# Attention pairs before two gated layers: scores moved ahead of all transposes, a second probability buffer, and weight splitting moved up in GpSimd's queue

## What is computed

```python
B, H, S, D = 4, 8, 576, 64
scores = where(causal, -1e9, q @ k.T / sqrt(D));  a = softmax(scores);  local = a @ v
q_p = phi(q)                                   # phi(x) = x > 0 ? x + 1 : exp(x)
mem_out = (q_p @ M_prev) / (q_p @ z_prev + 1e-6)
attn = g * mem_out + (1 - g) * local           # g = sigmoid(beta) by head
x = attn as 2304 tokens x 512
h = x @ w_in;  x = act(h) @ w_out              # 512 -> 2048 -> 512, piecewise quadratic gate
h = x @ w_in2; out = (h * sigmoid(h)) @ w_out2 # 512 -> 2048 -> 512
```

## Time and profile before

| | us |
|---|---|
| median of 3 runs | 986.52 (985.75 to 989.36) |
| the profiled execution | 986.77 |
| its span, first to last instruction | 984.6 |
| TensorE busy | 974.2 (99%) |
| VectorE, ScalarE, GpSimd busy | 478.4, 384.0, 286.0 |

### The profile page before, as it was taken

The page is one execution under the profiler, slowest core; times in us unless marked ns, Lnnn a source line. Parts: engine busy times, 40 slices in busy tenths (PEclk is TensorE's granted clock), DMA queues, the critical chain, the costliest instruction groups (busy, mean ns, idle before and its releaser), DMA issues.

```text
span 984.6 us, 14130 instructions
## 1 busy us (share of the span) xinstructions
PE 974.2 (99%) x5468; PEld 814.4 (83%) x5468; DVE 478.4 (49%) x946; ACT 384.0 (39%) x847; POOL 286.0 (29%) x304
## 2 busy tenths in 40 slices
PE   8999999999999999999999999999999999999998
PEld 6888778888888888888888998888888888888897
DVE  7999999756344434434344663323332332322232
ACT  7988888633223222322223332322222232222222
POOL 7999999799000000000000798000000000000000
PEclk9999999999999999999999999999999999999999
DMA  6555454244000000000000343001000100100010
GB/s 213 152 161 157 145 145 141 60 128 117 12 1 1 1 0 1 1 1 1 1 1 1 87 133 92 0 1 43 1 1 1 44 0 1 43 1 1 1 44 22
DMA packets 38401, 48.10 MB, mean 49 GB/s; under 512 B 3264, under 2 KB 21696, under 8 KB 38336
## 3 DMA queue, kind: packets, MB, share of 16 engines
q1 hardware_dynamic: 38336, 47.20, 16.0%
HBM read 42.47 MB, written 4.72 MB: 48 GB/s over the span
## 4 chain that ended last, share of the span: by engine, by line
PE 89%; DVE 6%; ACT 2%; issue 1%; DMA 0%; POOL 0%; SPq 0%; POOLq 0%
PE ps L1020 26%; PE ps L1022 26%; PE ps L1021 26%; PE ps L953 3%; PE ps L898 3%; PE ps L861 2%; DVE prob L652 1%; PE ps L973 1%; PE ps L877 1%; DVE glo L796 1%; ACT prob L475 1%; DVE qlo L634 1%; DVE rw L684 1%; PE ps L939 1%; PE ps L946 1%
## 5 line engine op out<-in xcount | busy, mean ns | idle before, releaser
L1020 PE MATMUL ps<-xhi,W 128*128 128x512 f32 (+1 forms) x640 | 235.5, 368 | 0.0
L1021 PE MATMUL ps<-xlo,W 128*128 128x512 f32 (+1 forms) x640 | 235.4, 368 | 0.0
L1022 PE MATMUL ps<-xhi,W 128*128 128x512 f32 (+1 forms) x640 | 235.4, 368 | 0.0
L796 DVE TENSOR_TENSOR glo<-act_t,ghi 128x512 fp32r<-128x512 f32 (+1 forms) x160 | 118.1, 738 | 223.5 <-ACT ghi L575 223.5
L575 ACT CAST ghi<-act_t 128x512 fp32r<-128x512 f32 (+1 forms) x160 | 92.5, 578 | 235.4 <-PE ps L1022 213.1
L1020 PEld LDWEIGHTS ps<-xhi,W 128*128 128x128 f32 x640 | 120.6, 188 | 20.7
L1021 PEld LDWEIGHTS ps<-xlo,W 128*128 128x128 f32 x640 | 120.6, 188 | 20.6
L1022 PEld LDWEIGHTS ps<-xhi,W 128*128 128x128 f32 x640 | 120.6, 188 | 20.0
L335 POOL CAST W<-stage 128x512 fp32r<-128x512 f32 x64 | 49.1, 767 | 303.0 <-PE ps L1022 300.6
L567 ACT ACTIVATE act_t<-act_t,half_col 128x512 f32<-128x512 f32 (+1 forms) x80 | 54.5, 681 | 185.7 <-DVE act_t L789 185.7
L1020 PE MATMUL ps<-ghi,W 128*128 128x512 f32 (+1 forms) x320 | 118.1, 369 | 0.2
(11 more groups left out here) (113 smaller groups left out, 1334.9 us busy)
## 6 DMA issues: line engine op xcount, KB each, us to landing
stage<-in_moe_w_in SPq DMA_DIRECT2D x32, 256.0 KB, 2.7
stage<-in_moe_w_out SPq DMA_DIRECT2D x32, 256.0 KB, 2.7
vn<-in_vN SPq DMA_DIRECT2D x16, 320.0 KB, 4.5
qraw<-in_qT SPq DMA_DIRECT2D x15, 320.0 KB, 3.4
qn<-in_qN SPq DMA_DIRECT2D x16, 288.0 KB, 4.1
zb<-in_zN SPq DMA_DIRECT2D x32, 144.0 KB, 3.8
out_x<-ostage SPq DMA_DIRECT2D x17, 256.0 KB, 2.0
kraw<-in_kT SPq DMA_DIRECT2D x15, 288.0 KB, 3.0
```

Of the source, the lines that this page charges most:

```text
L796: nc.vector.tensor_tensor(glo[:, f % SLOTS, 0:TN[tile]], a, ghi[:, f % SLOTS, 0:TN[tile]].bitcast(F32), ALU.subtract).then_inc(glo_done, 1)
L1020: nc.tensor.matmul(dst, w_lo_, x_hi_, start=first, stop=False)
L1021: nc.tensor.matmul(dst, w_hi_, x_lo_, start=False, stop=False)
L1022: return nc.tensor.matmul(dst, w_hi_, x_hi_, start=False, stop=last)
```

## The change

In its turn p (from p = 1 on) TensorE takes the four score blocks of pair p+1 first, straight behind the value products of pair p-1, and then all transposes of pair p. `prob` has two buffers, chosen by p % 2, so the maxima of pair p+1 need not wait until the blocks of pair p are turned. T_M0 is turned into bank 0, T_M30 into bank 1, T_M21 into bank 0 after T_M0 is emptied. VectorE's turn starts with `to_x(p-1)` and maxima 0 to 3, and only then has `rows(p)` and `empty_second(p)`. ScalarE makes the feature rows and three exponentials ahead of T_M0. GpSimd has `split_part` behind `widen(p)` and ahead of `phi_sum_2(p+1)`.

```diff
@@ -82,7 +82,7 @@
         phs = sb("phs", [P, NB + 1, D], where=att)
         vn = sb("vn", [P, 2, FULL + 1, 2, D], where=att)
         mb = sb("mb", [P, 2, P], where=att)
-        prob = sb("prob", [P, 2, tri(FULL) * P], where=att)
+        prob = sb("prob", [P, 2, 2, tri(FULL) * P], where=att)
         ptail = sb("ptail", [P, MAIN + P], where=att)
         probT = sb("probT", [P, 2, FULL + 1, S], where=att)
         turned = sb("turned", [P, 2, S], where=att)
...
@@ -430,6 +431,9 @@
                 weigh(p)
                 widen(p)
 
+                for u in parts_beside(p):
+                    split_part(u)
+
                 if 0 < p < NPAIR - 1:
                     phi_sum_2(p + 1)
                 if p + 2 < NPAIR:
...
@@ -438,8 +442,6 @@
                 if p + 1 < NPAIR:
                     phi_times_z(p + 1)
                     weigh_v(p + 1)
-                for u in parts_beside(p):
-                    split_part(u)
             for u in range(2 * EARLY, 4 * FC):
                 split_part(u)
 
...
@@ -521,27 +523,30 @@
                 more = p + 1 < NPAIR
 
                 made_here = p + 2 if p else 1
+                if p == 0:
+                    phi_part_1(1)
+                    empty_main(0, T_M20, 2, 0)
+                    empty_main(0, T_M30, 3, 0)
+                    phi_part_2(1)
+                elif made_here < NPAIR:
+                    phi_part_1(made_here)
+                    phi_part_2(made_here)
+                if more:
+                    for c in range(3):
+                        exps(p + 1, c)
                 if p:
                     empty_first(p)
-                if made_here < NPAIR:
-                    phi_part_1(made_here)
-                empty_main(p, T_M20, 2, 0)
-                if p == 0:
-                    empty_main(0, T_M30, 3, 0)
-                if made_here < NPAIR:
-                    phi_part_2(made_here)
                 if more:
-                    exps(p + 1, 0)
-                    exps(p + 1, 1)
+                    exps(p + 1, 3)
                 if p:
+                    empty_main(p, T_M20, 2, 0)
                     empty_main(p, T_M30, 3, 0)
-                if more:
-                    exps(p + 1, 2)
-                    exps(p + 1, 3)
+                if p and more:
+                    exps(p + 1, 4)
                 empty_main(p, T_M31, 3, 1)
                 empty_tail(p)
-                if more:
-                    exps(p + 1, 4)
+                if p == 0:
+                    exps(1, 4)
                 empty_rest(p)
                 empty_phi(p)
                 empty_row(p)
...
@@ -733,18 +734,17 @@
             dve.wait_ge(made, 14)
             for p in range(NPAIR):
                 more, more2 = p + 1 < NPAIR, p + 2 < NPAIR
+                if p and more:
+                    to_x(p - 1)
+                if more:
+                    for c in range(4):
+                        maximum(p + 1, c)
                 if p:
                     for step in range(4):
                         rows(p, step)
-                    if more:
-                        to_x(p - 1)
-                        empty_second(p)
-                    else:
-                        empty_second(p)
-                        to_x(p - 1)
-                if more:
-                    for c in range(4):
-                        maximum(p + 1, c)
+                    empty_second(p)
+                if not more:
+                    to_x(p - 1)
                 if p == 0:
                     norms(0, 0)
                     norms(0, 1)
...
@@ -850,8 +850,8 @@
                     pe.wait_ge(lo_done, 2 * p + 2)
                     if p:
                         pe.wait_ge(s_read, NB * p)
-                if s == 2 and p:
-                    pe.wait_ge(ev_act, len(BY_ACT) * (p - 1) + BY_ACT.index(T_M0) + 1)
+                if s == 2 and p == 1:
+                    pe.wait_ge(ev_act, BY_ACT.index(T_M0) + 1)
                 if s == 3:
                     pe.wait_ge(x_free, p)
                 for part, (a, b_) in enumerate(three_of):
...
@@ -868,9 +868,9 @@
                 if half == 0:
                     pe.wait_ge(s_read, NB * p + 4)
                     if p:
-                        pe.wait_ge(ev_act, len(BY_ACT) * (p - 1) + BY_ACT.index(T_M30) + 1)
+                        pe.wait_ge(ev_dve, len(BY_DVE) * (p - 1) + BY_DVE.index(T_M21) + 1)
                 elif p:
-                    pe.wait_ge(ev_dve, len(BY_DVE) * (p - 1) + BY_DVE.index(T_M21) + 1)
+                    pe.wait_ge(ev_act, len(BY_ACT) * (p - 1) + BY_ACT.index(T_M30) + 1)
                 at, _n = score_at(FULL, 0)
                 c = slice(half * HALF, (half + 1) * HALF)
                 for part, (a, b_) in enumerate(((qlo[i], khi[i]), (qhi[i], klo[i]), (qhi[i], khi[i]))):
...
@@ -881,10 +881,18 @@
 
             def room(p, u):
                 if u == T_M0:
-                    pe.wait_ge(s_read, NB * p + 5)
-                elif u in (T_M30, T_M21):
-
-                    pe.wait_ge(s_read, NB * (p + 1) + ((3 if u == T_M30 else 4) if p + 1 < NPAIR else 0))
+                    if p == 0:
+                        pe.wait_ge(s_read, 5)
+                    else:
+                        pe.wait_ge(s_read, NB * (p + 1) + (3 if p + 1 < NPAIR else 0))
+                elif u == T_M30:
+                    if p + 1 < NPAIR:
+                        pe.wait_ge(s_read, NB * (p + 1) + 4)
+                elif u == T_M21:
+                    if p == 0:
+                        pe.wait_ge(s_read, NB + 3)
+                    else:
+                        pe.wait_ge(ev_act, len(BY_ACT) * p + BY_ACT.index(T_M0) + 1)
                 elif u == T_REST:
                     if p + 1 < NPAIR:
                         pe.wait_ge(s_read, NB * (p + 1) + 6)
...
@@ -991,16 +999,16 @@
             pe.wait_ge(made, 14)
             for p in range(NPAIR):
                 more = p + 1 < NPAIR
-                turn_both(p, T_M0, 0)
-                turn_both(p, T_M1, 1)
-
-                if p:
-                    turn_corner(p)
+                if p == 0:
+                    turn_both(0, T_M0, 0)
+                    turn_both(0, T_M1, 1)
                 if more:
                     for s in range(FULL):
                         score(p + 1, s)
-                if p == 0:
-                    turn_corner(p)
+                if p:
+                    turn_both(p, T_M0, 0)
+                    turn_both(p, T_M1, 1)
+                turn_corner(p)
                 turn_one(p, T_M30, 3, 0)
                 turn_one(p, T_M21, 2, 1)
                 turn_one(p, T_M31, 3, 1)
```

More of the change, by code:

```diff
@@ L151, in build @@
         RING = [T_M1, T_M20, T_M31, T_TAIL, T_PHI, T_ROW]
-        AMONG_SCORES = {T_M0: 2, T_M30: 0, T_M21: 1, T_REST: 3}
+        AMONG_SCORES = {T_M0: 0, T_M30: 1, T_M21: 0, T_REST: 3}
         BY_ACT = [T_M0, T_M20, T_M30, T_M31, T_TAIL, T_REST, T_PHI, T_ROW]
@@ L157, in build @@
         LAST_BANK = {T_PHI: 0, T_ROW: 1}
-        LAST_PRIOR = {T_PHI: T_M30, T_ROW: T_M21}
+        LAST_PRIOR = {T_PHI: T_M21, T_ROW: T_M30}
         def ring(p, u):
@@ L164, in ring @@
                 return ps[:, 4 + RING.index(u) % 2, :]
-            return ps[:, AMONG_SCORES[u], :]
+            return ps[:, 2 if p == 0 and u == T_M0 else AMONG_SCORES[u], :]
         def emptied(p, u):
@@ L473, in exps @@
                 m, e = c // 2, c % 2
-                a = prob[:, e, tri(m) * P:tri(m) * P + keys(m)] if m < FULL else ptail[:, D:]
+                a = prob[:, p % 2, e, tri(m) * P:tri(m) * P + keys(m)] if m < FULL else ptail[:, D:]
                 nc.scalar.activation(a, a, ACT.Exp, bias=negmax[:, p % 2, c:c + 1], scale=-1.0,
@@ L639, in maximum @@
                 dve.wait_ge(s_full, UNITS * p + U_OF[m] + 1)
-                if (p, c) == (1, 4):
-                    dve.wait_ge(t_full, T_M20 + 1)
-                if p and c == 7:
-                    dve.wait_ge(t_full, TURNS * (p - 1) + T_M31 + 1)
                 at, n = score_at(m, e)
@@ L646, in maximum @@
                 if m < FULL:
-                    over, dst = mask[:, D + MAIN + P - n:], prob[:, e, tri(m) * P:tri(m) * P + n]
+                    over, dst = mask[:, D + MAIN + P - n:], prob[:, p % 2, e, tri(m) * P:tri(m) * P + n]
                 else:
@@ L897, in turn_block @@
                     c = (tri(m) + j) * P
-                    last = nc.tensor.transpose(ring(p, u)[:, at + j * P:at + (j + 1) * P], prob[:, e, c:c + P], ident[:])
+                    last = nc.tensor.transpose(ring(p, u)[:, at + j * P:at + (j + 1) * P], prob[:, p % 2, e, c:c + P], ident[:])
                 return last
```

## The result

The changed kernel took 993.12 us (992.17 to 994.38, 6 runs); the kernel before took 987.27 beside it (985.75 to 989.36, 6 runs). The ratio is 1.0062, with a 95% interval of 1.005 to 1.0074: slower by 0.6%. 992.3 was predicted. The profiled execution took 994.38, the slowest of the six. The mean granted clock was 1.000 in one of the six runs, at 992.17 us, and 0.998 in the other five.

The account below looks back on a forecast made before the run. In the attention stage a VectorE-GpSimd loop of 11.09 us a pair was to outlast TensorE's 10.96. Twelve loops plus 9.6 us for five weight pieces moved the layers' start from 192.10 to 197.7: plus 5.6, 992.3 us, range 989.3 to 995.5.

Parts of the forecast that it names:

- The joint of TensorE's new order: TensorE, value products to scores: counted as a switch of 0.09 us; three a pair for four, so 10.96 us a pair.
- The ring: Row weights through GpSimd's high parts, VectorE's `norms` and `to_x` to the next row weights: 11.09 us, setting the pair.
- `low_k` was to wait: VectorE's `low_k` waits for GpSimd's high part, some 0.8 us in nearly all turns 1 to 13, 2.7 in five.
- B: Rival: the ring is shorter than TensorE's pair, say 10.9 us; plain turns 10.96, time 990.0; chance 0.22.
- C: Rival: the ring is longer, by holds or late waits, 0.25 us in 12 turns, 995.3; chance 0.13.
- The piece: GpSimd's weight split ahead of `high_k`: 1.92 us in each of five turns, 9.6 us; TensorE waits for `qlo` and `X`.
- rival A: No ring: GpSimd has high parts ready in time, all TensorE waits go, 5.7 us less, 981.0; chance 0.07.
- the hold: VectorE's nine-element product in `rows` stands about 1 us until GpSimd's instruction ends; expected to vanish in the changed kernel.
- Rival D: The granted clock falls to 1.2 GHz for two microseconds after each of five waits, adding 5 us: 997; chance 0.03.
- ScalarE's first turn: Turn 1: feature rows come late as ScalarE makes two sets; TensorE may wait up to 0.6 us.
- The stage end: End of the attention stage, where the layers start: 197.7 us, where it was 192.10.
- R: Moment when a pair's row weights are ready: 3.05 us after TensorE leaves the value products.

Follow-up runs that it names:

- experiment 10: Changed kernel with `rows` ahead of the fourth maximum and weight pieces in turns 13, 14, 14 and five in turn 15: 986.27 us, ratio 1.0002.
- experiment 6: Changed kernel with the weight piece at the end of GpSimd's turn and `high_k`, `high_q` ahead of `phi_sum_2`: 989.12 us, ratio 1.0028.
- experiment 8: Changed kernel with `high_k`, `high_q` ahead of `phi_sum_2` and weight pieces in turns 13, 14, 14 and five in turn 15: 987.29 us, ratio 1.0004.
- experiment 5: Changed kernel with two weight pieces in each of turns 5, 9, 13 and 15, none in 7, 11 and 14: 998.68 us, ratio 1.0128.
- experiment 7: Changed kernel with weight pieces in turns 13, 14, 14 and five in turn 15: 989.2 us, ratio 1.002.
- Experiment 1: Changed kernel with the weight piece back at the end of GpSimd's turn: 988.23 us, ratio 1.0017.
- experiment 9: Kernel before with weight pieces in turns 13, 14 and six in turn 15, nothing else: 984.83 us, ratio 0.9985.
- experiment 12: Kernel of experiment 11 with the piece of turn 13 moved to the last turn, so one in 14 and seven in 15: 983.17 us, ratio 0.9961.
- experiment 2: Changed kernel with VectorE's `rows(p)` ahead of `to_x` and the four maxima: 988.96 us, ratio 1.0022.
- experiment 4: Kernel before with the weight piece behind `widen` and ahead of `phi_sum_2`, nothing else: 986.13 us, ratio 0.9997.
- experiment 11: Kernel of experiment 10 with weight pieces in turns 13, 14 and six in turn 15: 984.08 us, ratio 0.9978.

## Why the prediction was right

**The joint of TensorE's new order.** Predicted 0.09 us a pair and 10.96 in sum. Where TensorE sets the pace it is 10.98 (44.33 to 55.31 in the changed kernel, eleven turns in experiment 10), so one switch less is worth 0.07. By the rule of the Trainium skill in "TensorEngine Tiling (Array Packing)", Key Properties, the mode change drains the array. The traces agree as far as they go: a switch costs, 0.07 to 0.09 us. It was right to count the new joint as one.

**The ring.** Predicted 11.09 us; measured 11.07 in the mean of the twelve turns from `to_x` of turn 2 to that of turn 14, once pieces and clock are taken off (37.43 to 181.19 is 143.76; less 9.58 and 1.38, by 12). `low_k` was to wait 0.8 and 2.7 us: 0.74 and 2.65. Rivals B (shorter ring) and C (longer) are out; the margin against B was small, 0.08 us a pair, and experiment 10 shows how little it takes to turn it. One stretch was named too narrowly: the ring also closes through `phi_times_z` and `norms` (experiments 6 and 8). The number held, since it was taken from the start of `high_k` to the end of `norms` with all that lies in it.

**The piece.** Predicted 5 x 1.92 = 9.6 us: the five turns with a piece are 9.58 longer than plain ones. L336 and L338 run from 75.49 to 77.42, 1.93 us, so the piece suffers no hold. The rule of the Trainium skill in "SBUF — State Buffer", Who interferes with whom, which rival A cites, has it so: beside it VectorE has maxima, with one input in SBUF. Experiments 5 and 7 double and remove it: twice 1.92, and 1.92 each. Experiment 1 moves it out of the way of `high_k`, and half its cost stays, with the hold back in the ring. TensorE's weight loads wait 1.37 to 1.49 us for `qlo` in all five turns (1.4 predicted) and 0.6 for `X` (0.6).

**Rival A**, no ring, fell at once, by the second row of the wait sums. Its premise was right, that the holds of the earlier trace rows vanish: the nine-element product takes 0.17 us in all of turns 1 to 15. Only in turn 1 was `rows` held, at its first instruction (L674, 27.59, 0.73 us for 0.16). The holds had cost some 3.3 us (experiment 9), and the ring with its pieces takes more than it gives back.

**Rival D**, the clock, came true in one turn of five. The waits that it was to follow are 1.23 to 1.35 us in all five, and only the one in turn 6 was followed by a fall. The chance of 0.03 was for all five. But 0.998 in five of the six runs, where 21 of 31 runs of the kernel before are at 0.999 or more, says that some stretch at the lower clock is common here. Where it lies in the runs without a profile isn't on record, so the 1.3 us of the profiled execution above the median aren't explained by the fall that its profile shows.

**ScalarE's first turn.** Up to 0.6 us was allowed; the transposes of turn 1 wait 0.32 us for its T_M0 copy at 29.65.

**What was right only in sum.** The stage end was given as 197.7 where 199.90 less 1.4 for the clock is 198.5, 0.8 above. Half a microsecond lies ahead of turn 1 (25.47 for 24.95), and that is no property of the changed order: five kernels with the same turn 0 and full clock start turn 1 at 24.41, 24.91, 24.96, 25.02 and 25.22, and experiment 12 at 25.24. Another 0.45 is in turn 1, where R comes 3.50 us behind the first score for the 3.05 of the sum, with `rows` held as said. The median of the runs, 993.12, is also 0.8 above 992.3, but for other reasons: it has the lower clock in it, which the sum left out, and the kernel before took 987.27 in the median beside it, not the 986.52 or 986.77 from which the sum starts. The run at full clock, 992.17, is the one to compare. It is 6.1 us above the 986.08 of the kernel before at full clock, where 5.6 was predicted, and that it comes within 0.1 us of 992.3 is in part luck.

Two expectations of the experiments failed for a reason that the prediction also held: that a piece moved up frees `rows` from the hold. By itself it doesn't. The nine-element product takes 1.0 us with the piece early and `rows` early (experiments 2 and 4), and 1.08 with the piece last and `rows` late (experiment 1); of these kernels it is free only in the changed one, which has the piece early and `rows` late.

## What to carry to other kernels

Where an engine's in-order queue serves both something that arrives late and something that others need early, a delay of the first is passed on to the second; add up the ring of waits from one round to the next and compare it with the round of the engine that sets the pace. If the ring is the longer one, every instruction in it costs its full duration, background work above all, and a tenth of a microsecond of slack decides. Put background work into a round in which nobody waits for that queue: seven pieces in the last turn cost 0.9 us in all, behind the start of the layers, where one in a middle turn cost 1.9 us. And try such a move on the old order too, before the new order gets the credit (experiments 9 and 11).

## What the runs showed of the hardware

Behind turn 1, waits of 1.13 to 1.51 us of a busy TensorE were followed by a fall of the granted clock once in nine times (five in the changed kernel, two in experiment 7, one each in 8 and 10), waits of 3.2 us three times in three (experiment 5); each of these falls cost 0.9 to 2.3 us. Ahead of the first tail scores, at 9.5 to 10 us, where TensorE has other waits around, waits of 1.03, 1.22, 1.42 and 1.49 us were followed by a fall (experiments 5, 6, 8 and 7) and one of 1.13 us was not (the changed kernel). The wait alone doesn't tell whether the clock falls.

A product of 128 x 9 elements with both inputs in SBUF took 0.17 us alone and 1.0 us when GpSimd's instruction ran beside it (81.26 in experiment 4, 82.33 in experiment 2); both times it ended with GpSimd's. In these cases the one that starts later is the one that stands: in the changed kernel `high_q` starts first and keeps its 0.73 us, and `low_k`, 0.10 behind it, takes 1.24; in experiment 6 `low_k` starts first and takes 0.77, and `phi_sum_2`, 0.13 behind it, takes 1.83 where it otherwise takes 1.33.
